# Attention: one of six groups of small triangular blocks is inverted by VectorE, in the first pass, and not by GpSimd

## The reference, cut to what matters

```
y[t]  = r[t] @ state
Sa    = state @ a[t]
state = state * w[t] - outer(Sa, b[t]) + outer(v[t], k[t])
```

## Time and profile before

| | |
|---|---|
| median of 3 runs | 1255.68 us (1254.84 to 1255.77) |
| the profiled execution | 1257.5 us, its span 1255.4 us |
| first pass, DVE | 7.9 to 144.2 us |
| second pass | to about 442 us |
| POOL inverting | 43.3 to 348.6 us |
| PE, DVE, ACT, POOL busy, whole span | 998.0, 611.1, 287.8, 364.2 us |

### The profile page before, as it was taken

One profiled execution on the slowest core, in us unless ns is written; L12 is line 12 of the kernel. 1 busy time (PEld: TensorE's weight loads), 2 busy tenths in 40 slices (PEclk: granted clock), 3 DMA queues, 4 the chain that ended last, 5 costly groups with the idle time before them and its releaser, 6 DMA issues. The chain is left out here.

```text
span 1255.4 us, 43910 instructions
## 1 busy us (share of the span) xinstructions
PE 998.0 (79%) x19465; PEld 901.9 (72%) x19466; DVE 611.1 (49%) x943; ACT 287.8 (23%) x673; POOL 364.2 (29%) x465
## 2 busy tenths in 40 slices
PE   3432478887788855069999999995999999999998
PEld 2431478777778745058888888884888888898987
DVE  7995757666766656011111111113665646565654
ACT  4442334343344410000000001002212121212112
POOL 0598988988900020600042000004010100000000
PEclk9999988688887875579999999997999989999999
DMA  6755565776766440378877444542000000000000
GB/s 208 214 192 130 191 158 159 178 196 170 196 187 180 136 163 30 120 239 298 300 238 274 157 157 159 171 136 77 18 22 22 22 22 1 21 1 22 1 21 22
DMA packets 114472, 163.38 MB, mean 130 GB/s; under 512 B 58148, under 2 KB 87604, under 8 KB 113908
## 3 DMA queue, kind: packets, MB, share of 16 engines
q1 hardware_dynamic: 100004, 128.42, 33.8%
q0 software_dynamic: 5488, 24.13, 5.8%
q10 hardware_dynamic: 8928, 10.16, 2.3%
HBM read 131.98 MB, written 24.31 MB: 124 GB/s over the span
## 5 line engine op out<-in xcount | busy, mean ns | idle before, releaser
L814 PEld LDWEIGHTS h_bank<-xt,w 128*128 128x128 f32 x1488 | 172.7, 194 | 11.2 <-issue 6.4
L814 PE MATMUL h_bank<-xt,w 128*128 128x128 f32 x1488 | 173.0, 277 | 6.0 <-DMA w<-w_in 6.0
L844 DVE TENSOR_SCALAR ht<-h_bank 128x512 f32<-128x512 f32 x62 | 42.9, 692 | 273.7 <-PE h_bank L814 273.7
L126 POOL TENSOR_TENSOR solved<-solved,share 128x31 f32<-128x31 f32 (+15 forms) x186 | 138.1, 742 | 14.6
L827 PE MATMUL y_bank<-w_all,ht 128*128 x496 | 138.7, 433 | 1.6 <-DMA w_all<-w_in 1.6
L123 POOL TENSOR_TENSOR share<-solved,blk 128x31 f32<-128x31 f32 (+15 forms) x186 | 130.7, 703 | 14.6
L958 PE MATMUL y_bank<-w_out_hi,g_hi 128*128 128x320 f32 x384 | 121.5, 316 | 15.4 <-ACT y L1034 13.7
L1049 ACT CAST g_hi<-g 128x512 fp32r<-128x512 f32 x96 | 59.5, 620 | 301.8 <-DVE g L1010 301.8
L467 PE MATMUL bank<-alpha,second 40*64 40x64 f32 x1568 | 48.2, 284 | 98.7 <-DVE alpha L332 98.7
L958 PE MATMUL y_bank<-w_out_hi,g_lo 128*128 128x320 f32 x384 | 120.4, 314 | 0.0
L958 PE MATMUL y_bank<-w_out_lo,g_hi 128*128 128x320 f32 x384 | 120.2, 313 | 0.0
(11 more groups left out here) (145 smaller groups left out, 1640.8 us busy)
## 6 DMA issues: line engine op xcount, KB each, us to landing
w<-w_in SPq DMA_DIRECT2D x31, 1024.0 KB, 5.2
t_in<-wab_in SPq DMA_DIRECT2D x24, 776.0 KB, 6.2
t_in<-wak_in SPq DMA_DIRECT2D x24, 776.0 KB, 5.0
w_all<-w_in POOLq DMA_DIRECT2D x8, 1280.0 KB, 9.0
rr<-rr_in SPq DMA_DIRECT2D x24, 384.0 KB, 3.2
w<-w_in SPq DMA_DIRECT2D x31, 256.0 KB, 6.2
vt<-vt_in SPq DMA_DIRECT2D x24, 256.0 KB, 2.9
vtm<-vtm_in SPq DMA_DIRECT2D x24, 240.0 KB, 2.8
```

The costliest lines, as they stand in the source:

```text
L126: link(eng.tensor_tensor(rest, rest, part, ALU.subtract))
L814: last = pe.matmul(h_bank[s][f // FH][:, f % FH * ET:(f % FH + 1) * ET], w1[s][:, k, f * PARTS:(f + 1) * PARTS], xt[s][:, k, :], start=k = ...
L844: dve.tensor_scalar(ht[s][:, FH * n:FH * n + FH, :].rearrange("q f t -> q (f t)"), h_bank[s][n][:, :], 0.0, None, ALU.max).then_inc(s_relu, 1)
```

## The change

The group that DVE inverts is `BY_DVE` = 1; POOL does groups 0, 2, 3, 4 and 5. DVE runs `invert_blocks` on group 1 after the scaled inputs of step 11 of the first pass, with its own scratch tile and its own semaphore (`s_step_dve`), and goes on with step 12 afterwards. SP's stores and loads move: the store of group 0 and the load of group 2 from step 17 to step 16 of the first pass; the store of group 1 and the load of group 3 from step 1 of the second pass to step 17 of the first; the next two pairs from steps 5 and 9 to steps 4 and 8; the store of group 4 from step 13 to step 12; that of group 5 stays at 17.

```diff
--- before.py
+++ after.py
@@ -127,6 +127,8 @@
 
 
 INVERT_STEPS = 2 + 2 * (B - 1)
+BY_DVE = 1
+BY_POOL = [g for g in range(GROUPS) if g != BY_DVE]
 
 
 def attention(nc, inp, dram, keep):
@@ -156,7 +158,7 @@
         inv_in = ring("inv_in", 2, [PARTS, HS, B])
         w_tm, sa_tm, swt = (m_.sb(n, [PARTS, HS, DIM]) for n in ("w_tm", "sa_tm", "swt"))
         blk, solved = (ring(n, 2, [PARTS, B, B]) for n in ("blk", "solved"))
-        share = m_.sb("share", [PARTS, B * B // 4])
+        share, share_dve = (m_.sb(n, [PARTS, B * B // 4]) for n in ("share", "share_dve"))
         bank = [ctx.enter_context(nc.psum_tensor(f"bank{n}", [PARTS, 2, 512], F32)) for n in range(4)]
         BA, BB, BC, BD = bank
 
@@ -166,7 +168,7 @@
         s_wqx, s_inv_in, s_blk, s_tt, s_g1st = ([m_.sem(f"{n}{s}") for s in two] for n in (
             "s_wqx", "s_inv_in", "s_blk", "s_tt", "s_g1st"))
         s_ax, s_vt, s_vtm, s_rr = (m_.sem(n) for n in ("s_ax", "s_vt", "s_vtm", "s_rr"))
-        s_step = m_.sem("s_step")
+        s_step, s_step_dve = m_.sem("s_step"), m_.sem("s_step_dve")
         s_set, s_suf, s_rw, s_wq, s_wc, s_second, s_alpha1, s_alpha0, s_alpha = (m_.sem(n) for n in (
             "s_set", "s_suf", "s_rw", "s_wq", "s_wc", "s_second", "s_alpha1", "s_alpha0", "s_alpha"))
         names = ("g1", "bt", "w", "s", "u", "ktm", "z", "m1", "sa", "sat", "st", "g2", "m2", "y")
@@ -200,15 +202,21 @@
                 src = inp["wab"][j] if j < STEPS else inp["wak"][j - STEPS]
                 sp.dma_start(t_in[j % TR][:, :], src).then_inc(s_t[j % TR], 16)
 
+            def solved_group(g):
+                if g == BY_DVE:
+                    sp.wait_ge(s_step_dve, INVERT_STEPS)
+                else:
+                    sp.wait_ge(s_step, INVERT_STEPS * (BY_POOL.index(g) + 1))
+
             def load_blocks(g):
                 for s in two:
                     sp.wait_ge(s_g1st[s], 16 * GROUP // 2 * (g + 1))
                 if g >= 2:
-                    sp.wait_ge(s_step, INVERT_STEPS * (g - 1))
+                    solved_group(g - 2)
                 sp.dma_start(blk[g % 2][:, :, :], dram["g1"][g].rearrange("j b t -> b j t")).then_inc(s_blk[g % 2], 16)
 
             def store_inverses(g):
-                sp.wait_ge(s_step, INVERT_STEPS * (g + 1))
+                solved_group(g)
                 sp.dma_start(dram["tt"][g].rearrange("j b t -> b j t"), solved[g % 2][:, :, :]).then_inc(s_tt[g % 2], 16)
 
             def load_inverses(k):
@@ -262,9 +270,12 @@
                              g1s[k % 2][:, :, :].rearrange("q p t -> q (p t)")).then_inc(s_g1st[k % 2], 16)
                 if k in (5, 9):
                     load_blocks(k // GROUP - 1)
-                if k == 17:
+                if k == 16:
                     store_inverses(0)
                     load_blocks(2)
+                if k == 17:
+                    store_inverses(1)
+                    load_blocks(3)
                 if k == 20:
                     load_rr(0)
                     load_vtm(0)
@@ -278,10 +289,13 @@
                 more = k + 1 < STEPS
                 if k + TR < STEPS:
                     load_t(STEPS + k + TR)
-                if k % GROUP == 1 and k // GROUP + 1 < GROUPS:
-                    store_inverses(k // GROUP + 1)
-                    if k // GROUP + 3 < GROUPS:
-                        load_blocks(k // GROUP + 3)
+                if k in (4, 8):
+                    store_inverses(k // 4 + 1)
+                    load_blocks(k // 4 + 3)
+                if k == 12:
+                    store_inverses(4)
+                if k == 17:
+                    store_inverses(5)
                 if more:
                     cross_wq(k + 1)
                     load_vt(k + 1)
@@ -347,6 +361,9 @@
                 if k >= 1:
                     dve.wait_ge(did["bt"], k)
                 scaled(k, s_alpha1)
+                if k == 11:
+                    dve.wait_ge(s_blk[BY_DVE % 2], 16)
+                    invert_blocks(dve, s_step_dve, 0, blk[BY_DVE % 2], solved[BY_DVE % 2][:, :, :], share_dve[:, :])
             decays(STEPS)
             dve.wait_ge(did["bt"], STEPS)
             scaled(STEPS, s_alpha0)
@@ -388,11 +405,11 @@
         def _(pool):
             pool.memset(inv[:, :, :], 0.0)
             pool.memset(off[:, :, :], 0.0).then_inc(s_zero, 1)
-            for g in range(GROUPS):
+            for n, g in enumerate(BY_POOL):
                 pool.wait_ge(s_blk[g % 2], 16 * turn(g))
                 if g >= 2:
                     pool.wait_ge(s_tt[g % 2], 16 * turn(g - 2))
-                invert_blocks(pool, s_step, INVERT_STEPS * g, blk[g % 2], solved[g % 2][:, :, :], share[:, :])
+                invert_blocks(pool, s_step, INVERT_STEPS * n, blk[g % 2], solved[g % 2][:, :, :], share[:, :])
 
         @block.scalar
         def _(act):
```

## The result

The changed kernel is slower: 1268.68 us median of 4 runs (1266.91 to 1270.95) against 1255.71 (1254.84 to 1255.77), a ratio of 1.0106 with the 95% interval 1.0087 to 1.0125. A second set gave 1.0135 (1.0085 to 1.0185). The forecast was 1266, slower.

What follows compares the result with a forecast made beforehand. DVE was taken to bound the first pass, and a PE, ACT and DVE chain the second. First pass +17.8 and second -7.3 gave +10.5 on 1255.7, so 1266.2 us, range 1251 to 1275.

Steps and rivals of the forecast that it cites:

- DVE bounds the first pass, and the attention's loss is the whole effect: Later stages start behind a barrier after the attention, untouched, so its gain or loss counts one for one; forecast +10.5 us.
- The inversion by itself, 24.2 us: DVE's inversion of group 1 undisturbed: 62 operations in 23.0 us plus 1.2 for two memsets, ending at 85.6.
- Turns, T between 96.3 and 99.3, taken as 97.5: T is when DVE finishes its inversion; each DVE operation waits for one POOL operation until POOL ends group 0.
- SP's store at T + 24.5: SP stores group 0 after step 16's blocks, issued at T + 23.9 and taking 0.6; T is DVE's inversion end.
- The waits of steps 20 and 21, 3.5 and 3.1: First pass: DVE waits for inputs issued behind a store and load, 11.75 us after the store; together 0 to 10 us.
- a sign of being wrong: First pass: the forecast is wrong if DVE waits more than 10 us for inputs.
- Steps 21 to 24, 20.8: First pass: four steps at 5.2 us each beside POOL's group 2, completing the pass at 162.0, 17.8 us later.
- The second pass, -7.3: Gain of 6.3 us as step 1 loses its store and load, plus 1 us from less POOL beside DVE.
- the 1 us put down to POOL's shorter presence: Second pass: POOL beside DVE for about 50 us less is worth 1 us, 0 to 4.4.
- T below 91.5: Inversion end below which, without waits, the kernel is faster; stated in the rival where the cover holds, 1248.6, chance 0.14.

Runs made afterwards that it cites:

- A second set: The changed kernel run again with no edit: median 1269.08 us, ratio 1.0135 to the kernel before.
- the pair at 19: Changed kernel with the store of group 1 and load of group 3 at step 19 of the first pass, not 17: 1269.26 us, ratio 1.0149.
- the repeat: The changed kernel run again with no edit: median 1269.08 us, ratio 1.0135; waits before steps 20 and 21 of 3.80 and 5.67 us.
- the pair moved back: Changed kernel with store of group 1 and load of group 3 back at step 1 of the second pass: 1267.31 us, ratio 1.0135.
- changing 17 to 21: Kernel before with only the store of group 0 and load of group 2 moved from step 17 to 21 of the first pass: ratio 0.9967.
- the second alone: Kernel before with only second-pass stores (2, 6, 10, 14, 18) and loads (3, 7, 11) put in separate steps: 1241.94 us, ratio 0.9901.
- the kernel without group 0: Changed kernel with POOL only clearing group 0's tile and raising the semaphore, output wrong: one run, 1257.5 us.
- the changed kernel with its pairs split: Changed kernel with no store and load in one step (first pass 16 to 19; second pass stores 4, 8, loads 5, 9): 1262.11 us, ratio 1.0054.

## Why the prediction was right

Point by point, by its own steps:

- *DVE bounds the first pass, and the attention's loss is the whole effect.* Shown: +14.6 us at the end of the attention, +13.0 in the medians.
- *The inversion by itself, 24.2 us.* Measured 24.5 with POOL idle.
- *Turns, T between 96.3 and 99.3, taken as 97.5.* Measured 96.97. POOL ended group 0 at 90.31, inside the 89.7 to 92.7 worked out. The price of the turns is 11.0 us of the 35.4. Here lay the difference between no change and slower, and it came from two pairs of rows.
- *SP's store at T + 24.5.* Measured 121.53, T + 24.56.
- *The waits of steps 20 and 21, 3.5 and 3.1.* Measured 4.51 and 5.73. This is the term that was mis-sized, by 3.6 us in sum: the 11.75 us from the store to the scan were measured in the earlier trace rows on a queue that had been idle for 15 us. Here the same sequence took 134.40 - 121.53 = 12.9 the first time and 144.68 - 130.88 = 13.8 the second, with the backlog of the first behind it. The backlog as the reason for the second is argued from the order of the queue, not isolated: with the pair at 19, further away, 3.14 + 0.62 were left of the 5.73. The prediction allowed up to 10 us for both waits and named more than 10 as a sign of being wrong. They came to 10.2, so by that sign of its own it failed by a hair (9.5 in the repeat), while the path and the order of the waits held.
- *Steps 21 to 24, 20.8.* Measured 165.74 - 144.68 = 21.1. The pass: +21.5 against +17.8, and 3.6 of the 3.7 between them are the waits of steps 20 and 21.
- *The second pass, -7.3.* Measured -6.9 in the first profile and -3.1 in the repeat, so the size is confirmed only roughly. In both profiles the step from which the pair had gone took 11.1 us in place of 18.4, which is the whole of it; the 1 us put down to POOL's shorter presence no run tells apart, and no step of the pass waits for inverses. Where it came from is shown by the pair moved back: it is that pair's price, and the first pass paid it again as the wait of step 21. That the two would nearly cancel I had in the sum (3.1 against 6.3), but not as one thing.
- The time: 1266 forecast, 1268.7 measured. By the profiles 1268.0 against 1269.8: +3.7 in the first pass, +0.4 in the second, -2.7 in the stages that nothing touched, and 0.3 outside the span. That the total came so close is in part luck: the attention lost 14.6 us where 10.5 were forecast, and those 2.7 us hid the larger part of the 4.1 between them.
- One number of the rivals is off: *T below 91.5* as the limit of a faster kernel without waits. By the prediction's own terms the gain is nothing at T = 144.19 - 58.8 + 7.3 = 92.7 and 2.5 us at 90.2. Nothing hangs on it, since T came out at 96.97.

What the prediction did not use is that POOL's inversions were never what the attention waited for, except through SP's queue: the 21 us that POOL gained on group 0 brought nothing, and the same hole went by changing 17 to 21, at the price of 9.5 us in the step that then waited for the inverses.

## What to carry to other kernels

When an engine waits for a transfer, look first at what stands in front of it in the queue: moving the store and the load that blocked it, and not issuing two large transfers in one step, gave 1.6% here (1.0% the second alone), while giving the work to a second engine lost 1.1 to 1.3%. When a transfer is moved back, look also at who reads what it writes, and at what then stands behind it. Before work is moved to an engine that bounds its pass, price it at the pace that the engine has beside its neighbour (groups of the same shape with the neighbour idle and busy give it), not at its own.

## What the runs showed of the hardware

- DVE and POOL, both running chained operations on SBUF, took turns one for one (71.99 to 73.31 above), and did not share the loss evenly. Beside DVE's short operations POOL kept nearly its own pace (220 elements: 0.64 to 0.67 us, alone 0.61), and DVE was stretched from 0.42 to 0.69 us (252 elements); beside DVE's long scans the same POOL operation took 1.40.
- A DVE memset of 1024 elements took 0.91 us with POOL busy (61.53 after) and 0.91 with POOL idle (61.51 in the kernel without group 0), one case of each: it took no turns.
- With one transfer of 512 KB in pieces of 128 bytes just ahead of it, SP's issue of a load of 776 KB took 4.70 us when that was a store and 5.56 when it was a load (the changed kernel with its pairs split); the same issue took 0.34 at 101.19 in the changed kernel, after 36 us in which SP had issued nothing.
- The kernel before gave 1254.8 to 1255.8 us in one set of runs and 1242 to 1257 in the others. Among the latter the time tends to go with the mean granted clock of TensorE: 1256.6 us at 0.903, 1242.0 at 0.926.
